# A longer lag in an attention pipeline, transfers of two heads at a time, and normalising moved to GpSimd

## The reference, cut to what matters

```
# 2 batches, 8 heads, 768 positions, 64 per head; n_sink 4, window 128
scores = (q @ k.T) / sqrt(64)
keep   = (column < n_sink) | (0 <= row - column < window)
a      = exp(where(keep, scores, -1e9) - rowmax);  a = a / (a.sum(-1) + 1e-9)
x      = a @ v                                      # heads side by side: 1536 x 512
# layer 1: h = x @ w_in, softmax-gated, layer norm, @ w_out       (1536 x 512)
# layer 2: logits = x @ w_gate (8 experts), 8 Sinkhorn rounds, then
out    = sum over e of P[:, e] * (relu(x @ w1[e]) @ w2[e])
```

## Time and profile before

| | |
|---|---|
| median of 3 runs | 1267.88 us (1267.87 to 1268.62) |
| the profiled execution, own time | 1269.56 us |
| its span | 1267.8 us |
| TensorE busy, matmul | 1245.0 us, 98% |
| VectorE, ScalarE, GpSimd busy | 55%, 29%, 41% |
| first slices of 1/40 of the span, TensorE | 6, 8, 8, 9, then 9 to the end |
| granted clock in them | 8, then 9 (tenths, 9 is 90% or more) |

### The profile page before, as it was taken

How to read it: one execution, slowest core, us unless ns; L and a number is a source line. 1 busy time by engine, 2 the same in 40 slices (tenths; PEclk the granted TensorE clock), 3 DMA queues, 4 the chain that set the end, 5 groups by cost and what they waited for, 6 DMA issues and landing times.

```text
span 1267.8 us, 18739 instructions
## 1 busy us (share of the span) xinstructions
PE 1245.0 (98%) x6462; PEld 1099.8 (87%) x6462; DVE 692.3 (55%) x1347; ACT 362.7 (29%) x823; POOL 524.6 (41%) x576
## 2 busy tenths in 40 slices
PE   6889999999999999999999999999999999999998
PEld 4556899998998999999999999999999999999997
DVE  5885645345665555555555555555555555555554
ACT  5774534332224222222222222222222222222221
POOL 5553313553443444444444444444444444444441
PEclk8999999999999999999999999999999999999999
DMA  6661000011111111111111111111111111111102
GB/s 160 171 144 47 1 1 1 17 34 34 34 34 34 34 34 34 34 33 33 33 33 33 33 33 33 33 33 33 35 36 38 40 33 33 33 33 34 34 17 100
DMA packets 62800, 53.17 MB, mean 42 GB/s; under 512 B 9889, under 2 KB 50081, under 8 KB 62753
## 3 DMA queue, kind: packets, MB, share of 16 engines
q1 hardware_dynamic: 61888, 52.04, 14.4%
q10 hardware_dynamic: 864, 0.53, 0.2%
HBM read 49.40 MB, written 3.15 MB: 41 GB/s over the span
## 4 chain that ended last, share of the span: by engine, by line
PE 94%; DVE 2%; ACT 2%; SPq 1%; issue 1%; POOL 1%; DMA 0%; DVEq 0%; ACTq 0%
PE ps L743 30%; PE ps L744 29%; PE ps L745 29%; PE ps L715 1%; PE ps L689 1%; PE ps L793 1%; PE ps L669 1%; DVE pT L1229 1%; PE ps L721 1%; PE ps L926 1%; ACT acc L1156 1%; ACT probs L990 1%; POOL probs L510 1%; ACT xw L1009 0%; DVE xw L1239 0%
## 5 line engine op out<-in xcount | busy, mean ns | idle before, releaser
L1462 DVE SCALAR_TENSOR_TENSOR acc<-ps,gate_now,acc 128x512 f32<-128x512 f32 x336 | 252.2, 751 | 166.2 <-PE ps L745 163.3
L743 PE MATMUL ps<-ring 128*128 128x512 f32 x768 | 300.6, 391 | 0.0
L744 PE MATMUL ps<-ring 128*128 128x512 f32 x768 | 299.8, 390 | 0.0
L745 PE MATMUL ps<-ring 128*128 128x512 f32 x768 | 299.2, 390 | 0.0
L1138 ACT ACTIVATE sums<-ps 128x384 f32<-128x384 f32 x192 | 94.2, 491 | 598.0 <-PE ps L745 598.0
L1438 DVE TENSOR_TENSOR sums<-ps,sums 128x384 f32<-128x384 f32 x192 | 106.8, 556 | 158.3 <-ACT sums L1138 107.1
L745 PEld LDWEIGHTS ps<-ring 128*128 128x128 f32 x768 | 144.2, 188 | 30.9
L743 PEld LDWEIGHTS ps<-ring 128*128 128x128 f32 x768 | 144.2, 188 | 27.9 <-DVE acc L1458 0.4
L744 PEld LDWEIGHTS ps<-ring 128*128 128x128 f32 x768 | 144.2, 188 | 25.8
L591 POOL TENSOR_TENSOR w_raw<-w_raw 128x256 f32<-128x256 f32 x32 | 23.7, 740 | 322.9 <-PE ps L745 322.9
L743 PE MATMUL ps<-xw,ring 128*128 128x384 f32 x448 | 152.4, 340 | 0.3 <-ACT sums L1138 0.2
(11 more groups left out here) (140 smaller groups left out, 1760.5 us busy)
## 6 DMA issues: line engine op xcount, KB each, us to landing
w_in<-w_exp SPq DMA_DIRECT2D x64, 256.0 KB, 3.2
w_raw<-w_exp SPq DMA_DIRECT2D x64, 128.0 KB, 2.6
w_raw<-w_exp SPq DMA_DIRECT2D x32, 256.0 KB, 3.1
v_sb<-v SPq DMA_DIRECT2D x16, 192.0 KB
out<-acc SPq DMA_DIRECT2D x12, 256.0 KB, 2.0
q_sb<-qT SPq DMA_DIRECT2D x14, 192.0 KB, 4.3
k_sb<-kT SPq DMA_DIRECT2D x14, 192.0 KB, 4.5
k_sb<-kT SPq DMA_DIRECT2D x16, 128.0 KB, 4.2
```

The costliest lines, as they stand in the source:

```text
L743: pe.matmul(o, ws[0], xs[0], start=first, stop=False, skip_group_check=True)
L744: pe.matmul(o, ws[0], xs[1], start=False, stop=False, skip_group_check=True)
L745: return pe.matmul(o, ws[1], xs[0], start=False, stop=last, skip_group_check=True)
L1462: dve.scalar_tensor_tensor(out=acc[:, T, :], in0=y_bank(u, T), scalar=gate_now[:, T:T + 1], in1=acc[:, T, :], op0=ALU.mult, op1=ALU.add).t ...
```

## The change

- **Lag.** On TensorE `pv(p, 0)` moves from the pair's own last tile to the next pair's tile 1, `turn_sinks` to the same place ahead of it, `pv(p, 1)` to tile 3, and `pv(p, 2)` with `pv_sinks` to tile 5. ScalarE's and VectorE's work on a pair's result moves to tile 0 two pairs on. v is loaded later, ahead of the weights' piece.
- **Normalising.** GpSimd scales three tiles of each batch, ScalarE none. ScalarE copies the sinks' transposes.
- **Transfers.** q and k go by three transfers of 128 partitions for a pair. The sinks are copied to both ends of each block on chip: by VectorE for pair 0, by GpSimd (`lay_sinks`) for the others.
- **Logits.** A second copy of the gate's weights stands 64 columns on, so that one product with `B11` serves two blocks: 16 products of two parts (32 matmuls) instead of 20 (40).

```diff
@@ -98,6 +98,7 @@
 WG_AT = 32 * (NB - 1)
+WG_TWIN = 64
...
@@ -110,7 +111,7 @@
 q_sb = sb("q_sb", [P, 2, SEQ], F32, in_a)
-k_sb = sb("k_sb", [P, 2, QT - 1, PW], F32, in_a)
+k_sb = sb("k_sb", [P, 2, QT - 1, PW + NS], F32, in_a)
...
@@ -211,6 +212,7 @@
 qk_first, qk_second, qk_third = sem("qk_first"), sem("qk_second"), sem("qk_third")
+sinks_laid = sem("sinks_laid")
...
@@ -300,7 +302,7 @@
-ACT_USES, DVE_USES = (0, 2, 5), (1, 3, 4, 6)
+ACT_USES, DVE_USES = (0, 2, 4, 5), (1, 3, 6)
 def copied(p, use):
@@ -365,37 +367,29 @@
-def load_first_qk(queue, h):
-    rows_h = slice(64 * h, 64 * h + 64)
-    q_h, k_h = qT[0, h][0:DH], kT[0, h][0:DH]
-    n, at, front = 2 * P, h * NS, 3 * P
-    queue.dma_start(q_sb[rows_h, 0, 0:front], q_h[:, 0:front]).then_inc(qk_first, 16)
-    queue.dma_start(k_sb[rows_h, 0, 0, at:at + n], k_h[:, 0:n]).then_inc(qk_first, 16)
-    queue.dma_start(k_sb[rows_h, 0, QT // 2:QT - 1, at:at + n],
-                    k_h[:, P:SEQ - P].rearrange("d (a n) -> d a n", n=n)).then_inc(qk_second, 16)
-    sinks_at = (1 - h) * n
-    queue.dma_start(k_sb[rows_h, 0, :, sinks_at:sinks_at + NS],
-                    k_h[:, 0:NS].unsqueeze(1).to_broadcast([DH, QT - 1, NS])).then_inc(qk_second, 16)
-    queue.dma_start(q_sb[rows_h, 0, front:SEQ], q_h[:, front:SEQ]).then_inc(qk_third, 16)
-    queue.dma_start(k_sb[rows_h, 0, 1:QT // 2, at:at + n],
-                    k_h[:, n:SEQ].rearrange("d (a n) -> d a n", n=n)).then_inc(qk_third, 16)
+def sink_columns(p):
+    k_p = k_sb[:, p % 2, :, :]
+    ends = [k_p[:, :, at:at + NS] for at in (0, PW)]
+    return ends, k_p[:, 0:1, NS:2 * NS].to_broadcast([P, QT - 1, NS])
+def both_heads(a):
+    return a.rearrange("h r n -> (h r) n")[DH:3 * DH]
+q_0, k_0 = both_heads(qT[0]), both_heads(kT[0])
+FRONT = 3 * P
...
 def _(sp):
-    def load_qk(p, h):
-        rows_h = slice(64 * h, 64 * h + 64)
-        k_ph = kT[p, h][0:DH]
-        sp.dma_start(q_sb[rows_h, p % 2, :], qT[p, h][0:DH]).then_inc(qk_loaded[p % 2], 16)
-        at = h * NS
-        sp.dma_start(k_sb[rows_h, p % 2, 0:QT // 2, at:at + 2 * P],
-                     k_ph.rearrange("d (a n) -> d a n", n=2 * P)).then_inc(qk_loaded[p % 2], 16)
-        sp.dma_start(k_sb[rows_h, p % 2, QT // 2:QT - 1, at:at + 2 * P],
-                     k_ph[:, P:SEQ - P].rearrange("d (a n) -> d a n", n=2 * P)).then_inc(qk_loaded[p % 2], 16)
-        at = (1 - h) * 2 * P
-        sp.dma_start(k_sb[rows_h, p % 2, :, at:at + NS],
-                     k_ph[:, 0:NS].unsqueeze(1).to_broadcast([DH, QT - 1, NS])).then_inc(qk_loaded[p % 2], 16)
+    def load_qk(p):
+        k_p = both_heads(kT[p])
+        sp.dma_start(q_sb[:, p % 2, :], both_heads(qT[p])).then_inc(qk_loaded[p % 2], 16)
+        sp.dma_start(k_sb[:, p % 2, 0:QT // 2, NS:PW],
+                     k_p.rearrange("d (a n) -> d a n", n=2 * P)).then_inc(qk_loaded[p % 2], 16)
+        sp.dma_start(k_sb[:, p % 2, QT // 2:QT - 1, NS:PW],
+                     k_p[:, P:SEQ - P].rearrange("d (a n) -> d a n", n=2 * P)).then_inc(qk_loaded[p % 2], 16)
     def load_v(p, h):
...
@@ -407,9 +401,12 @@
-    load_first_qk(sp, 0)
-    for h in range(2):
-        load_qk(1, h)
+    sp.dma_start(q_sb[:, 0, 0:FRONT], q_0[:, 0:FRONT]).then_inc(qk_first, 16)
+    sp.dma_start(k_sb[:, 0, QT // 2:QT - 1, NS:PW],
+                 k_0[:, P:SEQ - P].rearrange("d (a n) -> d a n", n=2 * P)).then_inc(qk_second, 16)
+    sp.dma_start(k_sb[:, 0, 1:QT // 2, NS:PW],
+                 k_0[:, 2 * P:SEQ].rearrange("d (a n) -> d a n", n=2 * P)).then_inc(qk_third, 16)
+    load_qk(1)
...
@@ -421,15 +418,17 @@
             sp.wait_ge(scores_full, STEPS * (p - 1))
+            load_qk(p)
+        if p >= 3:
+            sp.wait_ge(x_full, p - 2)
             for h in range(2):
-                load_qk(p, h)
+                load_v(p - 1, h)
...
         load_segments(p)
-        if p >= 2:
-            sp.wait_ge(x_full, p - 1)
-            for h in range(2):
-                load_v(p, h)
+    sp.wait_ge(x_full, PAIRS - 2)
+    for h in range(2):
+        load_v(PAIRS - 1, h)
     def load_w1(u):
@@ -504,12 +503,20 @@
     def normalise(p, b):
         pool.wait_ge(norm_link, 2 * (BATCHES * p + b + 1))
-        for t in (2 * b, 2 * b + 1):
-            a = tile_probs(p, t, 1)
-            k = 2 * t + 1
+        for t, h, done in ((2 * b + 1, 0, probs_scaled), (2 * b, 1, None), (2 * b + 1, 1, probs_ready[1])):
+            a = tile_probs(p, t, h)
+            k = 2 * t + h
...
                                       ALU.mult)
-        last.then_inc(probs_ready[1], 1)
+            if done is not None:
+                last.then_inc(done, 1)
+    def lay_sinks(p):
+        pool.wait_ge(qk_loaded[p % 2], 48 * ((p + 1) // 2))
+        ends, sinks = sink_columns(p)
+        for a in ends:
+            last = pool.tensor_scalar(a, sinks, 1.0, 0.0, ALU.mult, ALU.add)
+        last.then_inc(sinks_laid, 1)
     def round_segments(j):
...
@@ -537,6 +544,8 @@
         normalise(p, 1)
+        if p + 1 < PAIRS:
+            lay_sinks(p + 1)
...
@@ -652,20 +661,22 @@
     def scores(p, t):
         if p == 0 and t == 0:
-            pe.wait_ge(qk_first, 64)
+            pe.wait_ge(qk_first, 32)
         if p == 0 and t == 2:
-            pe.wait_ge(qk_second, 64)
+            pe.wait_ge(qk_second, 16)
         if p == 0 and t == 3:
-            pe.wait_ge(qk_third, 64)
+            pe.wait_ge(qk_third, 32)
         if p > 0 and t == 0:
-            pe.wait_ge(qk_loaded[p % 2], 128 * ((p + 1) // 2))
+            pe.wait_ge(qk_loaded[p % 2], 48 * ((p + 1) // 2))
+        if t == 2:
+            pe.wait_ge(sinks_laid, p + 1)
...
             rows_h = slice(64 * h, 64 * h + 64)
-            w, at = width(t), k_from(t, h)
+            w, at = width(t), 0 if h == 1 and t >= 2 else NS
...
@@ -726,17 +737,17 @@
         if t == 1 and p > 0:
-            pv(p - 1, 1)
+            turn_sinks(p - 1)
+            pv(p - 1, 0)
         if t == 2 and p > 0:
-            turn_sinks(p - 1)
...
         if t == 3 and p > 0:
+            pv(p - 1, 1)
+        if t == 4:
+            turn(p, 0)
+        if t == 5 and p > 0:
...
             pv_sinks(p - 1)
-        if t == 4:
-            turn(p, 0)
-        if t == 5:
-            pv(p, 0)
     def three(o, ws, xs, first, last):
@@ -780,6 +791,7 @@
     back(PAIRS, 3)
+    back(PAIRS, 5)
     def turn_ln(b, f):
@@ -910,18 +922,15 @@
     def gate_logits():
-        pe.wait_ge(wg_ready, 2)
+        pe.wait_ge(wg_ready, 4)
...
         ops = []
-        for b in range(NB):
-            s = b // 2
+        for s in range(2):
             for c in range(2):
-                if b % 2 == 0:
-                    ops += [(b, s, c, B11, c), (b, s, 2 + c, B21, c)]
-                else:
-                    ops += [(b, s, c, B11, c), (b, s, c, T1, c), (b, s, 2 + c, B22, c)]
-        for n, (b, s, c, m, k) in enumerate(ops):
-            w = wg[:, c, WG_AT - 32 * b:WG_AT - 32 * b + P]
+                ops += [(0, s, c, B11, c), (0, s, 2 + c, B21, c), (1, s, c, T1, c), (1, s, 2 + c, B22, c)]
+        for n, (j, s, c, m, k) in enumerate(ops):
+            at = WG_AT - WG_TWIN * j - 32 * s
+            w = wg[:, c, at:at + P]
...
@@ -982,7 +991,8 @@
 def _(act):
-    load_first_qk(act, 1)
+    act.dma_start(k_sb[:, 0, 0, NS:PW], k_0[:, 0:2 * P]).then_inc(qk_first, 16)
+    act.dma_start(q_sb[:, 0, FRONT:SEQ], q_0[:, FRONT:SEQ]).then_inc(qk_third, 16)
     def exp_tile(p, k):
...
@@ -997,12 +1007,10 @@
-    def scale_probs(p, b):
-        act.wait_ge(norm_link, 2 * (BATCHES * p + b + 1))
-        a = tile_probs(p, 2 * b + 1, 0)
-        k = 4 * b + 2
-        act.activation(a, a, ACT.Copy, scale=a_stat[:, A_INV, k:k + 1]).then_inc(probs_scaled, 1)
+    def copy_sinkT(p):
+        act.wait_ge(pT_full, T_USES * p + SINK_USE + 1)
+        act.activation(sinkT[:, :], t_bank(p, SINK_USE)[0:2 * NS, 0:(QT - 2) * P],
+                       ACT.Copy).then_inc(pT_act, 1)
     def round_x(p):
...
@@ -1010,21 +1018,19 @@
     def back(p, t):
+        if t == 0 and p > 1:
+            round_x(p - 2)
...
             copy_pT(p - 1, 1, 0)
-            scale_probs(p - 1, 2)
-        if t == 2:
-            if p > 0:
-                copy_pT(p - 1, 2, 0)
-            scale_probs(p, 0)
+        if t == 1 and p > 0:
+            copy_sinkT(p - 1)
+        if t == 2 and p > 0:
+            copy_pT(p - 1, 2, 0)
...
             copy_pT(p, 0, 0)
-            scale_probs(p, 1)
...
         for t in range(QT):
-            if t == 4 and p > 0:
-                round_x(p - 1)
...
@@ -1032,6 +1038,8 @@
             act.activation(wg[:, :, WG_AT:WG_AT + EXPERTS], wg_raw[:, :, :], ACT.Copy).then_inc(wg_ready, 1)
+            at = WG_AT + WG_TWIN
+            act.activation(wg[:, 0:2, at:at + EXPERTS], wg_raw[:, 0:2, :], ACT.Copy).then_inc(wg_ready, 1)
@@ -1095,6 +1103,7 @@
     exp_h(0)
+    copy_sinkT(PAIRS - 1)
...
@@ -1229,10 +1238,6 @@
-    def copy_sinkT(p):
-        dve.wait_ge(pT_full, T_USES * p + SINK_USE + 1)
```

(27 more changed lines are left out.)

## The result

| | before | after |
|---|---|---|
| median | 1268.18 us (1267.87 to 1268.62, 4 runs) | 1257.84 us (1257.18 to 1258.79, 4 runs) |
| profiled execution, own time and span | 1269.56, 1267.8 us | 1257.18, 1255.4 us |
| TensorE, VectorE, ScalarE, GpSimd busy | 98, 55, 29, 41% | 99, 55, 28, 43% |
| one pair, tile-2 scores to tile-2 scores | 12.57 us | 11.41 us |
| first scores of pair 2 | 30.91 us | 26.64 us |

The ratio of after to before is 0.9917, 95% interval 0.9905 to 0.9928: faster by 0.83%. The forecast was 1257.3 us. Places are read from the profiled executions, totals from the medians.

The account below looks back on a forecast made before the run. TensorE was taken to bound the kernel, with GpSimd's batch 2 its new last wait. Terms -2.7 - 7.3 - 1.0 + 2.3 - 0.5 - 1.4 = -10.6 us gave 1257.3 us, own range 1254.5 to 1260, eight in ten 1252.5 to 1262.5.

Parts of the forecast that it names:

- The expected signs: Pair 11.2 to 11.6 us, one wait near 0.5, GpSimd over 9 us, `lay_sinks` under 0.3, pair 2 near 28.
- small waits on VectorE's port use: In GpSimd's stretch of the pair loop: an allowance of 0.33 us within its 5.58.
- Pairs, end and tail together: Attention: pairs 2 to 7 gain 7.3 us, last waits 1.0 and 0.5, less 2.3 of deferred work.
- the deferred 2.28: At pair 2's first scores, one batch's `pv` and `pv_sinks` more remain to do, 2.28 us paid back at the end.
- Logits: Logit matmuls at the end: eight fewer steps of 0.177 save 1.4 us on TensorE.
- Start: Up to pair 2's first scores: net -2.7 us, bounds 0 and -5.5, with the lower clock kept.
- loads of q and k: Transfers in attention: hidden before and after, with at least a microsecond of slack.
- So the 0.43 goes: TensorE's 0.43 us wait in a pair goes because ScalarE's sinks copy has a v product and score group as cover.
- the floor: TensorE's pair in attention without waits or drains: 10.84 us.
- rival 1: GpSimd's batch 2 ends 0.5 us earlier, pairs run at 10.84, six gain 3.1 more: about 1254; chance 0.20.
- Rival 2: GpSimd holds harder by slower `lay_sinks`, scalings or port blocking: pair 12.0 to 12.4, about 1262; chance 0.19.
- Rivals 3 and 4: 3: VectorE's queue holds pairs at 12.57, 1266 to 1268 (0.07, one other included); 4: GpSimd's loop passes 12.57, about 1270 (0.04).

Follow-up runs that it names:

- the two slower starts: Executions of the changed kernel with an extra GpSimd instruction where it idles (1260.46 us), and with 40 logit matmuls in place of 32 (1259.58 us).
- 40 logits: The changed kernel with 40 logit matmuls in place of 32; 1259.58 us, ratio 0.9930 to the kernel before.
- the kernel with the gate late: The changed kernel with the gate's weights rounded in pair 7 and subtracted behind the last x, not in pair 0; 1256.57 us.
- A head at a time: The changed kernel with q and k transferred for one head each again, the sinks still laid on chip; 1263.33 us.
- the kernel with two buffers: The changed kernel with two buffers for the pieces of w_in and w_out, GpSimd's rest of w_out behind batch 2's scaling; 1254.50 us.
- the two kernels with added work: The changed kernel with one unused 512-column GpSimd copy in pairs 1 to 7, inside its loop (1260.54 us) or where it idles (1260.46 us).
- the last kernel: The changed kernel with two buffers for the pieces, ScalarE's sinks copy ahead of tile 1's exps, and the gate's weights treated behind attention; 1252.79 us.

## Why the prediction was right, and where it was not

**What bounds.** Right: TensorE's chain, with waits in attention alone, and GpSimd's batch 2 as the new last wait. Loop 11.42 against 11.34, wait 0.37 against 0.5, `lay_sinks` 0.19 each. The expected signs came: pair in 11.2 to 11.6, no wait before products with v, 32 matmuls, GpSimd busy for 9.35 us of a pair, the lower clock near 20 us. The first scores of pair 2 were expected near 28 and came at 26.64 (28.12 and 28.17 in the two slower starts). The loop's 0.33 "for small waits on VectorE's port use" had no row behind it. What stands there is GpSimd's 0.33 from the end of the rest at 64.05 to batch 2 at 64.38, while VectorE ends its blocked statistic and inverts it.

**Terms.** Pairs, end and tail together: forecast -7.3 - 1.0 + 2.3 - 0.5 = -6.5, measured -6.51 - 0.05 = -6.56. The parts fit less well than their sum. The pairs gave 6 x 1.16 = 7.0. The stretch from the last pair's first scores to the first layer is 14.39 us before and 13.69 after, so 0.46 net was lost there where 1.3 was forecast: of the deferred 2.28 the 0.8 of `pv(7, 0)` is paid only behind the first layer's first products. Behind them 0.05 was gained where 0.5 was forecast, as the wait went but this product came in. Logits: -1.4, measured -1.42. Start: forecast -2.7, measured -4.27. The mis-sized term there is the second subtraction, taken at 1.2 and measured at 0.34 more than the single one (1.63 against 1.29), and with it the clock, which the forecast kept as before and which was lower for 3 us, not 6.5. In the execution with both subtractions blocked ("40 logits") the start is 28.17, 2.74 below before. The forecast described that case. Of the 1.53 between the two executions 0.53 is the later start of the sinks' transposes (19.70 against 19.17), and 1.0 the longer stretch at the lower clock.

**The total.** 0.5 us off, and part of that is luck: the sum missed the profiled difference by 12.4 - 10.6 = 1.8, while the two profiled executions stood 1.4 above and 0.7 below their medians.

**Wrong: loads of q and k.** The step says "Steady: hidden before and after" and "at least a microsecond of slack". In after the last transfer of k lands up to 5.8 us from its issue at 54.63, so at 60.4, and TensorE needs it at 60.87: some 0.4 of slack. The kernel with the gate late has one wait of 0.27 for it. SyncE's row, and its line's issue to landing:

```profile
54.63 0.61 SPq L391 DMA_DIRECT2D k_sb<-kT  x1
...
DMA to landing us min/median/max: 5.0/5.7/5.8
```

A head at a time the cover is gone, by 0.4 to 1.5 us in most pairs, and the whole is worth 4 to 5.5 us (by the spans and by the medians). I had read the loads as hidden at 12.57 a pair and not asked whether they would be at 11.4. The total held because the change contains both parts.

**Wrong: who copies the sinks.** "So the 0.43 goes" gave the credit to ScalarE. Without the lag the wait stays at 0.45, with VectorE's copy and the lag it is gone: the lag did it.

**Wrong: the floor, and rival 1.** With GpSimd's rest out of the loop a pair takes 11.18 and 11.15, not 10.84, and the floor without any wait is 10.98. Rival 1's time of 1254 was reached by the kernel with two buffers, but not its mechanism: by the spans the pairs gave 1.4 us there, where the rival had 3.1.

**Rival 2's mechanism was real, its size not.** A statistic is blocked once a pair, 0.69 in place of 0.17, not for a whole rest. In the two kernels with added work it is blocked for the whole of it, 1.26. The prediction's reading of VectorE's long scalings as blocking is borne out too: a 260-column scaling takes 0.82 here, and 0.36 in six pairs of the kernel with two buffers. Rivals 3 and 4 did not come: VectorE's queue waits for nothing of x's rest, and GpSimd's scalings step by 0.6.

## What to carry to other kernels

When a change shortens a period, price every hidden transfer again at the new period: what was covered at 12.6 us was late at 11.3, and the lag, worth 2 to 3 us alone, was worth 7 to 8 with the wide transfers in place. Walk the loop through all engines and ask for each queued instruction whether it stands ahead of one that the loop needs; putting one of GpSimd's rests behind a scaling was worth 2 to 3 us, at least as much as moving the scaling to another engine (2). An engine's idle time in a handshake is not spare time if its work can block the partner.

## What the runs showed of the hardware

- A VectorE instruction on 4 elements per partition (0.17 us alone) takes 1.26 us when GpSimd's 1.27 us rest starts just ahead of it.
- With q and k in transfers to 64 partitions the full queues moved 215 to 228 GB/s, with transfers to 128 partitions 369. Over 30 to 100 us the same bytes held the queues 1.3 times as long (62.7 against 47.6%).
- GpSimd's two copies of 20 elements per partition take 0.20 us each, hardly more than its instruction on one element (0.19).
- At the start TensorE's granted clock fell to 0.50, the 1.2 GHz level, by the end of waits of 1.25 and 2.26 us. In the last kernel, with waits of 0.93 and 2.12 us, it stayed at 1.00. The same eight products took 1.55 and 0.87 us.
